# Six attention matmuls of a unit, each alone between groups of three big matmuls

## The reference

```python
# q, k, v: (4, 8, 576, 64), fp32; causal attention in a window of 64 positions
scores = scale * q @ k.T
mask = (rel >= 0) & (rel < 64)
scores = where(mask, scores, -1e9) - max
attn = exp(scores) / (sum + 1e-09)
x = (attn @ v), heads side by side      # (2304, 512)
# layer 1, w_in (512, 2048), w_out (2048, 512)
h = x @ w_in;  x = maximum(0.01 * h, h) @ w_out
# layer 2, weights of its own
h = x @ w_in;  out = (h * cos(h)) @ w_out
```

## Time and profile before

| | |
|---|---|
| median of 3 runs | 912.01 us |
| lowest and highest | 910.81 and 912.53 us |
| profiled execution: its own time, which is its span from first to last instruction | 910.0 us |
| TensorE matmuls busy | 891.0 us, 98% |
| TensorE weight loads busy | 846.9 us, 93% |
| VectorE busy | 477.5 us, 52% |
| ScalarE busy | 393.2 us, 43% |
| granted TensorE clock | 1.000 over the whole span |

### The profile page before, as it was taken

How to read it: one execution, slowest core, us unless ns; L and a number is a source line. 1 busy time by engine, 2 the same in 40 slices (tenths; PEclk the granted TensorE clock), 3 DMA queues, 4 the chain that set the end, 5 groups by cost and what they waited for, 6 DMA issues and landing times.

```text
span 910.0 us, 14462 instructions
## 1 busy us (share of the span) xinstructions
PE 891.0 (98%) x5040; PEld 846.9 (93%) x5040; DVE 477.5 (52%) x1146; ACT 393.2 (43%) x978; POOL 83.9 (9%) x68
## 2 busy tenths in 40 slices
PE   6799999999999999999999999999999999999998
PEld 5799999999999999999999889998999999999997
DVE  6755555545555554555323555545545545545543
ACT  5566444433433343434345534434433434434433
POOL 2254300000000000000256400000000000000000
PEclk9999999999999999999999999999999999999999
DMA  8455322222221222220444300100200100100100
GB/s 279 136 168 177 113 77 64 64 84 63 63 71 64 76 63 73 60 67 0 142 116 139 116 1 0 69 0 0 69 0 0 69 0 0 69 0 0 36 1 36
DMA packets 36878, 59.72 MB, mean 66 GB/s; under 512 B 3952, under 2 KB 24816, under 8 KB 36848
## 3 DMA queue, kind: packets, MB, share of 16 engines
q1 hardware_dynamic: 36848, 59.33, 21.0%
HBM read 49.87 MB, written 9.44 MB: 65 GB/s over the span
## 4 chain that ended last, share of the span: by engine, by line
PE 94%; DVE 3%; ACT 1%; issue 1%; DMA 0%; SPq 0%; ACTq 0%; DVEq 0%
PE h_ps L305 43%; PE y_ps L330 22%; PE y_ps L337 21%; PE s_ps L265 3%; PE t_ps L292 3%; PE t_ps L280 1%; DVE probs L564 1%; DVE x_raw L577 1%; DMA qk_sb<-qk 0%; DVE probs L539 0%; DVE neg_max L546 0%; DVE row_sum L552 0%; ACT w_hi L400 0%; DVE act_in L598 0%; DVE probs L596 0%
## 5 line engine op out<-in xcount | busy, mean ns | idle before, releaser
L305 PE MATMUL h_ps<-x_hi,w_hi 128*128 128x384 f32 x768 | 264.0, 344 | 1.1 <-DVE g_raw L604 0.6
L305 PE MATMUL h_ps<-x_lo,w_hi 128*128 128x384 f32 x768 | 258.3, 336 | 0.0
L305 PE MATMUL h_ps<-x_hi,w_lo 128*128 128x384 f32 x768 | 257.6, 335 | 0.0
L305 PEld LDWEIGHTS h_ps<-x_hi,w_hi 128*128 128x128 f32 x768 | 144.7, 188 | 5.9 <-DVE g_raw L604 1.0
L305 PEld LDWEIGHTS h_ps<-x_hi,w_lo 128*128 128x128 f32 x768 | 144.5, 188 | 3.7
L305 PEld LDWEIGHTS h_ps<-x_lo,w_hi 128*128 128x128 f32 x768 | 144.2, 188 | 0.3 <-DVE x_lo L583 0.3
L610 DVE TENSOR_TENSOR g_lo<-g_raw,g_hi 128x384 fp32r<-128x384 f32 x192 | 107.2, 558 | 68.4 <-ACT g_hi L448 68.4
L448 ACT ACTIVATE g_hi<-g_raw 128x384 fp32r<-128x384 f32 x192 | 100.7, 524 | 93.9 <-DVE g_raw L604 56.1
L589 DVE TENSOR_TENSOR g_raw<-h_ps,act_in 128x384 f32<-128x384 f32 x96 | 53.5, 557 | 164.4 <-ACT act_in L430 164.4
L330 PE MATMUL y_ps<-g_hi,w_hi 128*128 128x384 f32 x384 | 134.1, 349 | 0.0
L430 ACT ACTIVATE act_in<-h_ps 128x384 f32<-128x384 f32 x96 | 47.1, 490 | 194.4 <-PE h_ps L305 194.4
(11 more groups left out here) (43 smaller groups left out, 961.0 us busy)
## 6 DMA issues: line engine op xcount, KB each, us to landing
qk_sb<-qk SPq DMA_DIRECT2D x72, 224.0 KB, 2.6
v_sb<-values SPq DMA_DIRECT2D x72, 128.0 KB, 2.1
w_raw<-w_in SPq DMA_DIRECT2D x32, 256.0 KB, 2.7
w_raw<-w_out SPq DMA_DIRECT2D x32, 256.0 KB, 2.9
layer_out<-y_out SPq DMA_DIRECT2D x6, 768.0 KB, 3.8
x_raw<-layer_out SPq DMA_DIRECT2D x6, 768.0 KB, 5.2
out<-y_out SPq DMA_DIRECT2D x5, 768.0 KB, 4.0
mask_sb<-mask SPq DMA_DIRECT2D x18, 128.0 KB, 2.1
```

The lines of the kernel that those rows point to most:

```text
L305: mm = pe.matmul(h_ps[j % 2][:, 0:CH], w[:, j, cols], x[:, kt, :], start=kt == 0 and a == 0, stop=kt == KT - 1 and a == 2)
```

## The change

The helpers of the three attention steps are split into halves, one matmul each; the first half carries the step's waits and the second raises its semaphore. In a slot, one half of `scores` now stands after the first block of three `up` matmuls, the other after the second block, one half of `transposes` after the third block, and the other after the fourth. `down` gets the halves of `values`: one after its third group of three, the other after its fourth. The order of the six is kept, no wait is added or dropped, and no other engine's program is touched. `down_done` is raised before the last half of `values`. The attention of chunk 0 keeps its order (its calls go through the halves, two in a row).

```diff
+            def scores_half(c, p, banks, a):
+                if a == 0:
+                    pe.wait_ge(qk_in[p % QRING], 16 * (UNITS // QRING * c + p // QRING + 1))
+                    if banks is later_banks:
+                        pe.wait_ge(scores_read, UNITS * c + p)
...
+            def transpose_half(c, p, banks, a):
+
+                if a == 0:
+                    if p == 0 and banks is first_banks:
+                        pe.wait_ge(ident_in, 16)
+                    pe.wait_ge(probs_done, UNITS * c + p + 1)
+                    if banks is later_banks:
+                        pe.wait_ge(o_copied, UNITS * c + p)
...
+            def values_half(c, p, banks, a):
+
+                if a == 0:
+                    pe.wait_ge(probsT_done, UNITS * c + p + 1)
...
             def chunk(n, layer, attends, last=False, next_layer=None):
                 for j in range(FT):
...
-                    if attends and j < UNITS:
-                        scores(n + 1, j, later_banks)
-                    if not (last and j + LEAD >= FT):
...
-                        up(*ahead)
+                        up(*ahead, range(0, 1))
+                    if attends and j < UNITS:
+                        scores_half(n + 1, j, later_banks, 0)
+                    if has_up:
+                        up(*ahead, range(1, 2))
+                    if attends and j < UNITS:
+                        scores_half(n + 1, j, later_banks, 1)
+                    if has_up:
+                        up(*ahead, range(2, 3))
                     if attends and 1 <= j <= UNITS:
-                        transposes(n + 1, j - 1, later_banks)
+                        transpose_half(n + 1, j - 1, later_banks, 0)
+                    if has_up:
+                        up(*ahead, range(3, 4))
+                    if attends and 1 <= j <= UNITS:
+                        transpose_half(n + 1, j - 1, later_banks, 1)
                     if not late:
-                        down(n, j, layer)
-                    if attends and 1 <= j <= UNITS:
-                        values(n + 1, j - 1, later_banks)
+                        down(n, j, layer, (n + 1, j - 1) if attends and 1 <= j <= UNITS else None)
```

and in `down`:

```diff
+                        if m == KT - 1 and not final:
+                            mm.then_inc(down_done, 1)
+                        if attend and m >= KT - 2:
+                            values_half(*attend, later_banks, m - (KT - 2))
```

More of the change, by code:

```diff
@@ L254, in _ @@
         def _(pe):
[L255 to L261, removed]
+            def scores_half(c, p, banks, a):
[3 more added lines that the diff above has]
+                        pe.wait_ge(scores_read, UNITS * c + p)
+                    elif p >= 2:
+                        pe.wait_ge(scores_read, p - 1)
@@ L262, in scores @@
                 s = banks[0][p % len(banks[0])]
                 u = qk_sb[:, p % QRING, :]
-                for a in range(2):
-                    mm = pe.matmul(s[:, P * a:P * a + P], u[:, P * a:P * a + P],
-                                   u[:, QC + TILE * a:QC + TILE * a + P], start=True, stop=True)
-                mm.then_inc(scores_done, 1)
-            def transposes(c, p, banks):
[L271 to L278, removed]
-                for a in range(2):
-                    mm = pe.transpose(t[:, P * a:P * a + P], probs[:, p % PRING, P * a:P * a + P], ident_sb[:])
-                mm.then_inc(transposed, 1)
@@ L283, in values @@
[L283 to L288, removed]
+                mm = pe.matmul(s[:, P * a:P * a + P], u[:, P * a:P * a + P],
+                               u[:, QC + TILE * a:QC + TILE * a + P], start=True, stop=True)
+                if a == 1:
+                    mm.then_inc(scores_done, 1)
@@ new lines, in scores @@
+            def scores(c, p, banks):
+                for a in range(2):
+                    scores_half(c, p, banks, a)
+            def transpose_half(c, p, banks, a):
[5 more added lines that the diff above has]
+                        pe.wait_ge(o_copied, UNITS * c + p)
+                    elif p >= 2:
+                        pe.wait_ge(probsT_done, p - 1)
+                t = banks[1][p % len(banks[1])]
+                mm = pe.transpose(t[:, P * a:P * a + P], probs[:, p % PRING, P * a:P * a + P], ident_sb[:])
+                if a == 1:
+                    mm.then_inc(transposed, 1)
@@ L289, in values @@
+            def transposes(c, p, banks):
+                for a in range(2):
+                    transpose_half(c, p, banks, a)
+            def values_half(c, p, banks, a):
+                if a == 0:
+                    pe.wait_ge(probsT_done, UNITS * c + p + 1)
+                    pe.wait_ge(v_in[p % VRING], 16 * (UNITS // VRING * c + p // VRING + 1))
+                    if banks is first_banks and p >= 2:
+                        pe.wait_ge(o_copied, p - 1)
                 o = banks[2][p % len(banks[2])]
@@ L290, in values @@
                 v = v_sb[:, p % VRING, :]
+                mm = pe.matmul(o[:, P * a:P * a + P], v[:, P * a:P * a + P], probsT[:, p % 2, P * a:P * a + P],
+                               start=True, stop=True)
+                if a == 1:
+                    mm.then_inc(pv_done, 1)
+            def values(c, p, banks):
                 for a in range(2):
-                    mm = pe.matmul(o[:, P * a:P * a + P], v[:, P * a:P * a + P], probsT[:, p % 2, P * a:P * a + P],
-                                   start=True, stop=True)
@@ L294, in values @@
-                mm.then_inc(pv_done, 1)
+                    values_half(c, p, banks, a)
             def up_part(n, j, kt):
@@ L308, in up_part, with up, down @@
                     mm.then_inc(up_done, 1)
-            def up(n, j):
-                pe.wait_ge(g_raw_done, FT * n + j - 1)
-                for kt in range(KT):
+            def up(n, j, kts=range(KT)):
+                if kts[0] == 0:
+                    pe.wait_ge(g_raw_done, FT * n + j - 1)
+                for kt in kts:
                     up_part(n, j, kt)
-            def down(n, j, layer):
+            def down(n, j, layer, attend=None):
                 tile = FT * n + j
@@ L340, in down @@
                             mm.then_inc(last_banks_done, 1)
-                if not final:
-                    mm.then_inc(down_done, 1)
+                    if not final:
+                        mm.then_inc(down_done, 1)
             def chunk(n, layer, attends, last=False, next_layer=None):
@@ L347, in chunk @@
                     late = j == FT - LEAD
+                    has_up = not (last and j + LEAD >= FT)
                     if late:
                         down(n, j, layer)
-                    if attends and j < UNITS:
-                        scores(n + 1, j, later_banks)
-                    if not (last and j + LEAD >= FT):
+                    if has_up:
                         if j + LEAD < FT:
```

## The result

The changed kernel takes 914.59 us (median of 9 runs, 913.78 to 915.38), the kernel before 912.53 us in the same rounds (910.81 to 913.10): a ratio of 1.0025 with a 95% interval of 1.0016 to 1.0033. That is slower by 2.1 us by the medians and 2.3 us by the ratio, twice the 1.1 us forecast, and 914.59 us lies inside the range of 910.6 to 916.7 us. The profiled execution took 914.65 us with a span of 912.8 us.

What follows compares the result with a forecast made beforehand. TensorE's own sequence was taken as the bound, matmuls busy for 98% of the span. Terms -0.5 + 1.6 = +1.1 us on a 912.0 us median gave 913.1 us; own range 911.4 to 914.5 us, 80% range 910.6 to 916.7 us.

Steps and rivals of the forecast that it cites:

- Pieces and their exposed loads: On TensorE each small piece exposes the one weight load behind it: 0.22 us a pair, 0.11 us a lone transposing piece.
- lone pieces get cheap: Rival: loads exposed at group edges vanish in part, 0.05 us saved in four more groups in 60 units, 901 us; 7%.
- The group term: Regrouping the small pieces on TensorE saves 0.01 us in each of 50 slots, -0.5 us, bounds 1.2 us up or down.
- the stream price: Rival: a piece at a group's end costs more than one inside; 0.008 us per end needed for 2 us, 915 us; 3%.
- The `o_copied` wait of slots 2 to 11: Transposing load waiting for the values copy: slack 0.80 us falls to 0.16 us, 0.04 to 0.09 after the message; no stall.
- The `o_copied` wait of slot 12: Slack of 0.35 us becomes -0.28 us; matmul 0.29 to 0.34 us late in five chunks, taken as 1.6 us.
- The rival in which this wait is absorbed: Slack in slot 12 is larger than read, no stall, only the -0.5 us stays: 911.5 us; 5%.
- `probs_done` in slot 1: Transposing load's wait for normalised probabilities: slack 0.59 us loses 0.52 us, 0.07 us remain against 0.05 us needed; no cost.
- the waits of `values` and `scores`: Values load keeps over 0.5 us of its 1.20 us slack, scores are needed later than before; no cost.
- every slot waits: Rival: message, queue and refill at the `o_copied` wait exceed 0.22 us; each missing 0.1 us costs 5 us, 918.6 us; 17%.

Runs made afterwards that it cites:

- r1: Changed kernel, but slot 12's two transposing matmuls together behind `up` as before: 912.67 us, ratio 1.0002 to before; five chunks 401.02 us, -0.13 us.
- r10: Changed kernel with slot 12's transposing matmuls together behind `up`, run once more for a second trace: 913.20 us; five chunks +0.97 us against before.
- r4: Changed kernel with the first transposing matmul one big `up` matmul earlier in every slot with transposes: 916.76 us, ratio 1.0046 to before.
- r2: Kernel before, but in slot 12 alone the first transposing matmul ahead of the last three of `up`: 912.66 us, ratio 1.0008.
- r9: Changed kernel, but in slot 12 alone the first transposing matmul one big matmul later: 913.35 us, one run.
- r7: Kernel before, with only the first transposing matmul moved ahead of the last three of `up` in every slot with transposes: 913.54 us, ratio 1.0013.
- r6: Changed kernel with the first transposing matmul two big `up` matmuls earlier: 926.12 us, ratio 1.0151 to before.

## Why the prediction was right, and where its sum was off

- *Pieces and their exposed loads*: right to 0.01 us. A pair costs 0.22 us and a lone piece 0.11 us wherever they stand. No edge gave a discount, so the rival "lone pieces get cheap" fell. The Trainium skill (TensorE: Matmul & The Clock Gate, section "Back-to-back issue gap") gives 81 ns for each 128-column matmul in a sustained stream of loads and matmuls; the trace disagrees, with 0.11 us a piece in rows of eight too.
- *The group term, -0.5 us with 1.2 us either way*: this is the term that was mis-sized, and its sign was wrong. The five chunks with the stalls taken off grew by 2.0 - 1.5 = 0.5 us in both traces of the changed kernel. That is 1.0 us over the forecast, and the stalls were 0.1 us under theirs, so the term is all of the miss. Two things were in it. A group more costs about 0.005 us, just what the prediction had allowed for the rounding of its rows, and always upward. And runs of big matmuls behind a small group have a short and a long form 0.03 us apart, for which the term had no room. The rows could have told: twelve big matmuls took 2.11 us behind the transposes and 2.08 us behind the scores, and I priced all of them at 2.08 / 12. r1 and r10, one order of instructions, stand at -0.13 and +0.97 us. That the sum kept within its bounds is in part luck: in the changed kernel the first effect was offset by the loss of the second in half of the slots.
- *The rival "the stream price"*: its mechanism, a cost at a group's end, is there, at 0.005 us where it asked for 0.008 us. Its 915 us lies nearer to the measured 914.59 us than the forecast's 913.1 us.
- *The `o_copied` wait of slots 2 to 11, 0.04 to 0.09 us of slack left to the load*: right, at its lower end. There was no stall: in the changed kernel the load starts 0.145 to 0.176 us behind the end of the copy, and where it is late it starts 0.115 us behind it, so 0.03 to 0.06 us were left. r4, one big matmul earlier, made the load late in every slot.
- *The `o_copied` wait of slot 12, taken as 1.6 us*: right, five times 0.29 to 0.30 us, 1.5 us. The rival in which this wait is absorbed fell with it. Two deviations worked against each other: the message took 0.12 us, at the upper end of its bounds, and the lateness that costs nothing is 0.11 us and not 0.06 us, since the load behind a late load follows at once. r1 (stall gone), r2 (stall alone, 0.19 us), r9 (one big matmul later, 0.12 us) and r7 show the cause from four sides.
- *`probs_done` in slot 1, and the waits of `values` and `scores`*: no new idle time at them in the main loop.
- *The rival "every slot waits"*: did not come about, but r6 shows its mechanism and price. Once the loop sets the pace, one more big matmul inside it costs its full time in each slot, 10.5 us in all.
- *The range and the chances*: the forecast's own range of 911.4 to 914.5 us ends just under the measured 914.59 us; against the 912.53 us of the kernel before in the same rounds, and not the 912.0 us of the forecast, the rise of 2.1 to 2.3 us is inside it. Its lower bound takes off 1.7 us, where its stated terms give 1.2 + 0.15 us. Within 0.2% was given 63%; the ratio of 1.0025 lies just past that line, and its interval on both sides of it.

Whether the wait itself could be removed was not tried: transposes and values share a bank, the kernel uses the other seven for something else, and VectorE still reads the values from it when TensorE would write the next transposes. Why a run takes the long form stays open. It is only shown that the order alone does not decide it, that a chunk mostly keeps its pattern of long and short slots, that the granted clock is 1.00 with either, and that in a long and a short slot of the changed kernel (slots 4 and 6 of chunk 0) the instructions of ScalarE and VectorE start within 0.01 us of the same place.

## What to carry to other kernels

Splitting small pieces up among big ones cost little in itself here, 0.02 us a slot, since each piece's exposed load goes with it. So price the waits that a moved piece carries: take the slack of each wait, subtract what the wait is moved ahead by and what its producer's chain is moved back by, and look at the first and last slots of a loop apart. Here only the slot without scores had too little slack, and it made three quarters of the loss. A wait in a loop through other engines was free while the loop was the shorter one; once it was the longer one, the next step inside it counted in full (r4, r6). And when two forms of the same run differ by more than the effect that is looked for, compare short with short and long with long: the totals of r1 and of the kernel before, 401.02 and 401.15 us, would have told that the split is free.

## What the runs showed of the hardware

- A small fp32 piece of 128 columns costs 0.11 us alone, in pairs and in rows of eight alike; each further group of them among big matmuls costs about 0.005 us more. The Trainium skill (TensorE: Matmul & The Clock Gate, section "LDWEIGHTS (loading the stationary operand)") gives 107 ns for a load of 128 columns, and the trace agrees.
- A weight load behind a late weight load starts 0.03 to 0.07 us after it, not 0.17 us. By the second load behind it 0.11 us are made good, so that much lateness in front of a lone piece is free (r4, r9, slot 12 of the changed kernel).
- The wait for `o_copied`, released through TensorE's sequencer, let the load start 0.12 us after its producer's end in every stall; at another place such a wait took 0.07 us, and a load that carries its wait itself 0.05 us.
- A run of nine big matmuls behind a small group took 1.56 to 1.57 or about 1.59 us in one and the same order, at a granted clock of 1.00, and two executions of one kernel differed in this by 1.1 us (r1, r10).
